# All six r scalings on VectorE, r's first scaling moved up in its slot, and the weight splits moved

## The reference, cut to what matters

```python
def _attn_ref(r, k, v, w, u):
    state = zeros(B, H, D, D)
    for t in range(S):
        cur = einsum('bhd,bhe->bhde', u * k[t], v[t])
        y[t] = einsum('bhd,bhde->bhe', r[t], state + cur)
        state = w[t][..., None] * state + einsum('bhd,bhe->bhde', k[t], v[t])

def _moe_ref(x, w_in, g_ln, w_sg, b_sg, w_out):
    h = gelu_tanh(x @ w_in)
    u, v = split(h)                      # halves of the columns
    v_n = layer_norm(v) * g_ln
    gated = u * (einsum('ts,bsd->btd', w_sg, v_n) + b_sg)
    return x + gated @ w_out

def _moe2_ref(x, mu_k, mu_r, w_k, w_v, w_r):
    xk, xr = mixes of x and x shifted by one step
    return sigmoid(xr @ w_r) * (relu(xk @ w_k) ** 2 @ w_v)
```

## Time and profile before

| | us |
|---|---|
| median of 3 runs (lowest, highest) | 423.65 (422.62, 425.02) |
| the profiled execution, its own time | 422.52 |
| its span | 420.8 |
| PE busy in the span | 368.8 (88%) |
| DVE busy | 260.1 (62%) |
| ACT busy | 182.2 (43%) |
| POOL busy | 125.0 (30%) |
| L565, r scalings on POOL, 24 instructions of 1762 ns | 42.2 |
| L870, r scalings on DVE, 16 of 1207 ns | 19.3 |
| L863, k scalings on DVE, 40 of 949 ns | 37.9 |
| L853, first_r on DVE, 16 of 569 ns | 9.1 |
| L1124, idle time of PE just before the w transposes | 22.6 |

### The profile page before, as it was taken

The page is one execution under the profiler, slowest core; times in us unless marked ns, Lnnn a source line. Parts: engine busy times, 40 slices in busy tenths (PEclk is TensorE's granted clock), DMA queues, the critical chain, the costliest instruction groups (busy, mean ns, idle before and its releaser), DMA issues.

```text
span 420.8 us, 9110 instructions
## 1 busy us (share of the span) xinstructions
PE 368.8 (88%) x3836; PEld 347.9 (83%) x3836; DVE 260.1 (62%) x380; ACT 182.2 (43%) x312; POOL 125.0 (30%) x141
## 2 busy tenths in 40 slices
PE   4656758879697899949999999999999999999997
PEld 3445647667596787849998999999999999999996
DVE  6467889797979983571645535998796311764011
ACT  3644627364554544543312406626783800565100
POOL 5936535271625732100000000520970000473000
PEclk9887869698888999959999999999999999999999
DMA  7997281716202101100100000305000011000011
GB/s 133 195 259 156 48 202 47 162 50 113 58 4 58 31 3 30 30 2 20 47 2 0 0 2 4 147 0 176 33 2 0 2 37 58 19 2 0 19 39 56
DMA packets 58840, 23.59 MB, mean 56 GB/s; under 512 B 52912, under 2 KB 56368, under 8 KB 58800
## 3 DMA queue, kind: packets, MB, share of 16 engines
q1 hardware_dynamic: 58800, 23.02, 22.1%
HBM read 18.29 MB, written 2.36 MB: 49 GB/s over the span
## 4 chain that ended last, share of the span: by engine, by line
PE 78%; issue 8%; ACT 6%; DVE 5%; SPq 1%; DMA 1%; POOL 0%; DVEq 0%; ACTq 0%; POOLq 0%
PE ps L1201 20%; PE ps L1202 19%; PE ps L1203 19%; PE ps L1192 4%; PE ps L1124 4%; PE ps L1188 3%; PE ps L1146 3%; PE ps L1134 2%; DVE kT L863 1%; PE ps L1157 1%; ACT ktok L651 1%; DVE sc L908 1%; PE ps L1129 1%; ACT rU L630 1%; ACT r L633 1%
## 5 line engine op out<-in xcount | busy, mean ns | idle before, releaser
L565 POOL TENSOR_TENSOR r<-r,wb 112x768 f32<-112x768 f32 x24 | 42.2, 1762 | 83.1 <-PE ps L1192 82.4
L613 POOL TENSOR_TENSOR sq_f<-sq_f 128x384 f32<-128x384 f32 x32 | 33.8, 1071 | 74.9 <-ACT sq_f L753 74.8
L863 DVE TENSOR_TENSOR kT<-kT,wb 112x384 f32<-112x384 f32 x40 | 37.9, 949 | 19.0 <-PE ps L1192 18.9
L1192 PE MATMUL ps<-r,kT 112*64 112x64 f32 x960 | 38.9, 238 | 7.1 <-DVE kT L863 4.3
L1192 PEld LDWEIGHTS ps<-r,kT 112*64 112x64 f32 x960 | 34.5, 150 | 12.7 <-issue 6.8
L1039 DVE TENSOR_TENSOR ot<-ps,ee 128x384 f32<-128x384 f32 x12 | 6.7, 558 | 54.6 <-PE ps L1203 54.6
L1024 DVE TENSOR_TENSOR sq_l<-sq_f,sq_h 128x384 fp32r<-128x384 f32 x32 | 27.7, 864 | 10.4 <-ACT sq_h L758 10.4
L1203 PE MATMUL ps<-xk_h,wk_l 128*128 128x384 f32 x96 | 32.2, 335 | 0.0
L1202 PE MATMUL ps<-xk_l,wk_h 128*128 128x384 f32 x96 | 32.2, 335 | 0.0
L1201 PE MATMUL ps<-xk_h,wk_h 128*128 128x384 f32 x96 | 32.2, 335 | 0.0
L1201 PE MATMUL ps<-wv_h,sq_h 128*128 128x384 f32 x96 | 32.1, 334 | 0.0
(11 more groups left out here) (146 smaller groups left out, 971.2 us busy)
## 6 DMA issues: line engine op xcount, KB each, us to landing
tok_w<-in_w_dram SPq DMA_DIRECT2D x16, 144.0 KB, 3.2
tok_k<-in_k_dram SPq DMA_DIRECT2D x16, 144.0 KB, 3.2
tok_r<-in_r_dram SPq DMA_DIRECT2D x16, 144.0 KB, 3.2
sgn<-in_moe_w_sg_dram SPq DMA_DIRECT2D x6, 384.0 KB, 3.9
vt<-in_v_dram SPq DMA_DIRECT2D x32, 72.0 KB, 2.6
out_dram<-ot SPq DMA_DIRECT2D x12, 192.0 KB, 1.9
xT<-yT SPq DMA_DIRECT2D x12, 144.0 KB, 2.6
win_raw<-in_moe_w_in_dram SPq DMA_DIRECT2D x1, 1536.0 KB, 7.5
```

Of the source, the lines that this page charges most:

```text
L565: nc.gpsimd.tensor_tensor(t, t, pair_of(h, 0, q).unsqueeze(1).unsqueeze(3).broadcast_to([ROWS, 2, S // (2 * h), h]), ALU.mult).then_inc(r_ ...
L613: nc.gpsimd.tensor_tensor(t, t, t, ALU.mult).then_inc(k_sq, 1)
L863: nc.vector.tensor_tensor(t, t, pair_of(h, 1, q).unsqueeze(2).broadcast_to([ROWS, S // (2 * h), h]), ALU.mult).then_inc(k_scaled, 1)
L1192: ins = nc.tensor.matmul(level_bank(l)[CHUNK[g], c * CH:(c + 1) * CH].rearrange("p (x t) -> p x t", x=2), kT[q % 4][0:ROWS, s], right2(r2[ ...
```

## The change

The level-3, level-4 and level-5 scalings of r leave GpSimd and stand in VectorE's list, each between scale_k and take_level of its level; GpSimd keeps the joins. Every wait on r_scaled_pool becomes one on r_scaled_dve. first_r and first_k are issued where their job stands in TensorE's order, so first_r comes after the old pair's level 5 and ahead of levels 3 and 1. low_sg and its semaphore go: ScalarE copies the sg transpose as plain fp32 to wsg_f (the same place as wsg_l), which alone frees the turn banks, and the six pieces of w_sg are split later from SBUF, cast by ScalarE in slots 15 to 18 and subtracted by VectorE in slots 16 to 19. The six w_in pieces move to slots 2 to 5 (cast) and 3 to 6 (low half), the three w_out pieces to slots 20 and 21. Up to slot 11 the low halves stand at the start of a slot, from slot 12 on after its levels and chain.

```diff
     for slot in range(SLOTS):
-        R_SCALES += [(q, l) for q, l in level_jobs(slot) if 0 < l < DVE_R]
         R_SCALES += [(q, 0) for kind, q, *_ in side_jobs(slot) if kind == "r"]
-    POOL_SCALES = [(q, l) for q, l in LEVEL_JOBS if l >= DVE_R]
+        R_SCALES += [(q, l) for q, l in level_jobs(slot) if l]
...
-    SPLITS = {2: ("in", 0), 3: ("in", 1), 4: ("in", 2), 5: ("in", 3), 6: ("in", 4), 7: ("in", 5),
-              15: ("out", 0), 16: ("out", 1), 17: ("out", 2)}
-    LOW_SLOTS = [3, 4, 5, 6, 7, 8, 20, 20, 21]
+    HIGH_SLOTS = {("in", 0): 2, ("in", 1): 2, ("in", 2): 3, ("in", 3): 4, ("in", 4): 4, ("in", 5): 5,
+                  ("sg", 0): 15, ("sg", 1): 16, ("sg", 2): 16, ("sg", 3): 17, ("sg", 4): 17, ("sg", 5): 18,
+                  ("out", 0): 20, ("out", 1): 20, ("out", 2): 21}
+    LOW_SLOTS = {("in", 0): 3, ("in", 1): 3, ("in", 2): 4, ("in", 3): 5, ("in", 4): 5, ("in", 5): 6,
+                 ("sg", 0): 16, ("sg", 1): 17, ("sg", 2): 17, ("sg", 3): 18, ("sg", 4): 18, ("sg", 5): 19,
+                 ("out", 0): 21, ("out", 1): 21, ("out", 2): 21}
...
@@ gpsimd @@
-            def scale_r(q, l):
-                h = 1 << l
-                pool.wait_ge(scores, level_at(q, l) + 1)
...
-                t = right2(r2[q % 5][0:ROWS, :, :], h)
-                nc.gpsimd.tensor_tensor(
-                    t, t, pair_of(h, 0, q).unsqueeze(1).unsqueeze(3).broadcast_to([ROWS, 2, S // (2 * h), h]),
-                    ALU.mult).then_inc(r_scaled_pool, 1)
...
             for slot in range(SLOTS):
-                for q, l in level_jobs(slot):
-                    if l >= DVE_R:
-                        scale_r(q, l)
                 for q, l in joins(slot):
                     join(q, l)
@@ scalar @@
-                    nc.scalar.copy(wsg_h[:, :, q * P:(q + 1) * P].rearrange("p (b j) t -> p b j t", b=2),
+                    nc.scalar.copy(wsg_f[:, :, q * P:(q + 1) * P].rearrange("p (b j) t -> p b j t", b=2),
...
+            def high_half(piece):
+                kind, n = piece
+                _, raw, hi = halves(piece)
+                if kind == "sg":
+                    act.wait_ge(copied, turn_at[("sg", C - 1)] + 1)
+                else:
+                    act.wait_ge(win_in if kind == "in" else wout_in, 16)
+                nc.scalar.copy(hi, raw).then_inc(w_high, 1)
...
+                for piece in PIECE_LIST:
+                    if HIGH_SLOTS[piece] == slot:
+                        high_half(piece)
@@ vector @@
-            def low_sg(n):
-
-                dve.wait_ge(copied, turn_at[("sg", n)] + 1)
...
             for slot in range(SLOTS):
+                for n, piece in enumerate(PIECE_LIST):
+                    if LOW_SLOTS[piece] == slot and slot < 2 * LEVELS:
+                        low_half(n)
                 for job in pe_jobs(slot):
                     if job[0] == "level":
                         q, l = job[1:]
                         if l:
                             scale_k(q, l)
-                        if 0 < l < DVE_R:
+                        if l:
                             scale_r(q, l)
                         take_level(q, l)
-                    elif job[0] == "sg":
-                        low_sg(job[1])
-                for job in side_jobs(slot):
-                    if job[0] == "k":
-                        first_k(job[1])
                     elif job[0] == "r":
                         first_r(job[1])
-                    elif job[0] == "u":
+                    elif job[0] == "k":
+                        first_k(job[1])
+                for job in side_jobs(slot):
+                    if job[0] == "u":
                         chain(job[1])
...
+                for n, piece in enumerate(PIECE_LIST):
+                    if LOW_SLOTS[piece] == slot and slot >= 2 * LEVELS:
                         low_half(n)
@@ tensor @@
-                elif last[0] == "sg":
-                    pe.wait_ge(sg_low, last[1] + 1)
...
-                    if l <= DVE_R:
-                        pe.wait_ge(r_scaled_dve, r_at(q, l - 1))
-                    else:
-                        pe.wait_ge(r_scaled_pool, pool_r_at(q, l - 1))
+                    pe.wait_ge(r_scaled_dve, r_at(q, l - 1))
...
-                        pe.wait_ge(sg_low, C)
+                        pe.wait_ge(w_low, split_at("sg"))
```

More of the change, by code:

```diff
@@ L115, in join_at @@
         return JOINS.index((q, l)) + 1
-    SPLITS = {2: ("in", 0), 3: ("in", 1), 4: ("in", 2), 5: ("in", 3), 6: ("in", 4), 7: ("in", 5),
-              15: ("out", 0), 16: ("out", 1), 17: ("out", 2)}
-    LOW_SLOTS = [3, 4, 5, 6, 7, 8, 20, 20, 21]
-    PIECES = len(SPLITS)
+    HIGH_SLOTS = {("in", 0): 2, ("in", 1): 2, ("in", 2): 3, ("in", 3): 4, ("in", 4): 4, ("in", 5): 5,
[4 more added lines that the diff above has]
+                 ("out", 0): 21, ("out", 1): 21, ("out", 2): 21}
+    PIECE_LIST = list(HIGH_SLOTS)
+    PIECES = len(PIECE_LIST)
     def split_at(kind):
-        return max(n + 1 for n, piece in enumerate(SPLITS.values()) if piece[0] == kind)
+        return max(n + 1 for n, piece in enumerate(PIECE_LIST) if piece[0] == kind)
     def segments(q):
@@ L171, in rwkv_gmlp_channel_mix_kernel @@
         wsg_l = at("wsg_l", [P, C, S], F32R, A_sg + SG)
+        wsg_f = at("wsg_f", [P, C, S], F32, A_sg + SG)
         A_out = A_sg + 2 * SG
@@ L403, in halves @@
                 return win_l[:, m, c], win_raw[:, m, c], win_h[:, m, c]
+            if kind == "sg":
+                return wsg_l[:, n, :], wsg_f[:, n, :], wsg_h[:, n, :]
             return [t.ap().rearrange("p f d -> p (f d)")[:, n * FH:(n + 1) * FH] for t in (wout_l, wout_raw, wout_h)]
@@ L542, in join @@
                         pool.wait_ge(k_scaled, k_at(q - 2, l + 1))
-                        if l + 1 < DVE_R:
-                            pool.wait_ge(r_scaled_dve, r_at(q - 2, l + 1))
-                        else:
-                            pool.wait_ge(r_scaled_pool, pool_r_at(q - 2, l + 1))
+                        pool.wait_ge(r_scaled_dve, r_at(q - 2, l + 1))
                     nc.gpsimd.tensor_tensor(blocks(q, 2 * h), pair_of(h, 0, q), pair_of(h, 1, q),
@@ L916, in low_half @@
             def low_half(n):
-                lo, raw, hi = halves(list(SPLITS.values())[n])
+                lo, raw, hi = halves(PIECE_LIST[n])
                 dve.wait_ge(w_high, n + 1)
                 nc.vector.tensor_tensor(lo, raw, hi.bitcast(F32), ALU.subtract).then_inc(w_low, 1)
-            def low_sg(n):
-                dve.wait_ge(copied, turn_at[("sg", n)] + 1)
-                c = slice(n * P, (n + 1) * P)
-                nc.vector.tensor_tensor(wsg_l[:, :, c].rearrange("p (b j) t -> p b j t", b=2),
-                                        turn[:, :, 0:HF].rearrange("p b (j t) -> p b j t", j=3),
-                                        wsg_h[:, :, c].bitcast(F32).rearrange("p (b j) t -> p b j t", b=2),
-                                        ALU.subtract).then_inc(sg_low, 1)
             def low_x(b, m):
@@ L1064, in _ @@
                         nc.vector.memset(aT[s][:, :, :, :], 0.0).then_inc(zeroed, 1)
-                for n in range(PIECES):
-                    if LOW_SLOTS[n] == slot:
+                for n, piece in enumerate(PIECE_LIST):
+                    if LOW_SLOTS[piece] == slot and slot >= 2 * LEVELS:
                         low_half(n)
@@ L1153, in y_job @@
                 pe.wait_ge(masked, level_at(q, LEVELS - 1) + 1)
-                pe.wait_ge(r_scaled_pool, pool_r_at(q, LEVELS - 1))
+                pe.wait_ge(r_scaled_dve, r_at(q, LEVELS - 1))
                 for n in range(1, NCH):
```

10 lines of the change are left out of this document (1 added, 9 removed).

## The result

| | before | changed |
|---|---|---|
| median, us (lowest to highest) | 424.33 (422.62 to 425.53) | 401.56 (400.33 to 402.79) |
| ratio, 95% interval | | 0.9466 (0.9417 to 0.9516) |
| profiled execution, its span | 420.8 | 398.7 |
| busy: PE, DVE, ACT, POOL | 368.8, 260.1, 182.2, 125.0 | 361.1, 259.8, 186.6, 87.2 |

The kernel is 22.8 us faster by the medians; 406.0 was forecast. VectorE is busy for as long as before, though it has taken over GpSimd's 24 multiplies.

The account below looks back on a forecast made before the run. VectorE and TensorE waiting for each other, through first_r's bank gate, were taken to bound the loop; 11.8 + 2.4 + 2.4 + 1.6 - 1.3 = 16.9 off 422.5 gives 405.6, median put at 406.0; range 401 to 417.

Parts of the forecast that it names:

- The bank gate and the low clock bound the kernel: Per period, TensorE's w transpose waits 2.08 us for first_r to free the turn banks, then runs slow at clock 0.85.
- the rival of the low clock: TensorE stays at slow prices and reaches the scan at 16.7 us, 1.7 above 15.0; time about 411.5, chance 0.20.
- VectorE's own work, 13.4 us a period: VectorE in one period: 12.3 us without GpSimd, less 1.5 for sg and w_in, plus 2.6 for three r scalings.
- Joins cost 1.2 and waits 0.35: Added to VectorE's 13.4 us for GpSimd's remaining joins and for waits, giving a period of 15.0 us.
- The rate of 0.42 us for each us of GpSimd: VectorE's stretch in the old period from 84.87: 3.4 us laid to GpSimd's 8.08 us busy.
- The rival of costly joins: GpSimd's joins cost VectorE their full length, up to 3.5 us, period 17.3; time about 414, chance 0.12.
- k waited for low_sg only another 0.5: On TensorE in the old period, k waited for low_sg until 101; freeing the sg transpose by ScalarE's copy saves 0.5 us.
- The stretch ahead of the first scan: 2.4 and 1.6: Gains of 2.4 us from 39.61 to 65.76 and 1.6 before 39.61, the latter bounded by 0 and 3.9.
- 1.3 us lost at the norm: Cost on the path of work not spread around the layer norm and of later ScalarE work; bounds 0 and 5.1.
- the cover: VectorE's 3.83 us wait for ScalarE at the norm's first low part, covering 3.5 us of work around the norm.
- VectorE slower through the contended price: Rival: moved scalings cost 2.27 us each whoever causes the long rows, period 20.2; time about 430, chance 0.08.
- The condition: The slower-VectorE rival decides from a period of 18.9 us on, that is from 5.5 us above 13.4.

Follow-up runs that it names:

- the fillers: Changed kernel with added GpSimd multiplies on a scratch tile in slots 7 to 14: 12 of 112x768 (long), 411.4 us, or 36 of 112x192 (short), 400.9 us.
- weights where they were: Changed kernel without its third part, w_sg split from PSUM in its own slot, w_in and w_out pieces where they were: 413 us by the ratio.
- after_again: The changed kernel itself, measured again beside the interleaved kernel: 402.2 us, ratio 0.9457.
- short fillers: Changed kernel with 36 added GpSimd multiplies of 112x192 on a scratch tile in slots 7 to 14: 400.9 us.
- ktok_first: Changed kernel with ScalarE's six casts of the normalised v behind the last pair's k transpose copy and wm copy: 399.8 us, ratio 0.9461.
- level 5 on GpSimd: Changed kernel with only level 5's scaling of r (8 of the 24) given back to GpSimd: 401.0 us, ratio 0.9467.
- the interleaved kernel: Changed kernel with last pair's k copy before the norm's casts, slot 20's gelus and state copy between them, last scan between norm steps: 392.5 us, ratio 0.9244.

## Why the prediction was right, and where it was not

The side was right and 401.56 lies near the low end of the range; the move was 22.8 us by the medians where 17.6 was forecast. The sum itself gave 405.6 for an execution like the profiled one and so 406.7 for the median; the 406.0 that was put down instead is not worked out. The low end of 401 stood on 13.9 us a period (measured 13.87) and no cost at the norm (measured 2.1). That the time comes within 0.6 of it all the same is in part luck: the early slots gave 1.8 more than their term and the stretch past the last u 0.6. By its steps:

- *The bank gate and the low clock bound the kernel.* The gate is shown: with first_r moved alone 14 us went and w follows kt at once. The clock over the three periods is 1.00 in that kernel and in the changed one, so the rival of the low clock does not hold. What the low clock cost by itself is not separated: with the scalings alone it rises to 0.97 and 12 us go though the gate stays. VectorE's stretched list was a limit beside the gate.
- *VectorE's own work, 13.4 us a period.* Right: 13.87 was measured, with VectorE full.
- *Joins cost 1.2 and waits 0.35.* This is the step that failed, by size: what is left beside 13.4 is 0.45, with no waits, and 0.33 of it is the one k multiply of 0.88. The rate of 0.42 us for each us of GpSimd came from long scalings, and the fillers show that short instructions do not cost it. Over the three periods it is the 3.4 us between 45.0 and 41.6. The rival of costly joins falls for the same reason.
- *k waited for low_sg only another 0.5.* The price fitted the old layout alone. In the new one the gate is 2.1 to 3.1 us a period, with the low clock behind it (weights where they were). The sum was not touched, since the change removes it; my picture of the third part as small was wrong.
- *The stretch ahead of the first scan: 2.4 and 1.6.* Measured 4.2 and 1.6, in one execution; the changed kernel reached the first scan 0.7 later in after_again. The early slots gain nearly a full period's gain in spite of the three low halves. That VectorE, at 21.40 of 21.97 busy, had no room left is shown; that the casts did not delay it is read from the trace, not tested.
- *1.3 us lost at the norm.* Measured 2.1, and for other reasons. The wait for ScalarE shrank from 3.83 to 1.17, so the cover held. What was lost is ahead of it: the u of slot 16 started 9.11 us behind the scan for 8.97 but ran at the low clock (2.47 for 1.48), and that of slot 18 waited 1.19 for its copy, behind two w_sg casts, for 0.81. With short fillers the first ran at 1.48 and the next u stood 25.6 us behind the scan, for 27.2 in the changed kernel and 25.3 before. Why the clock fell there stays open.
- *VectorE slower through the contended price.* The condition was never met: r multiplies average 974 ns.

What I had not seen at all is that the three parts are no sum. By the ratios, times 424 us, scalings alone give 11.6, first_r alone 13.2, the weights nothing; scalings with first_r 10.8, scalings with the weights 13.9, first_r with the weights 20.4; all three 22.6. Differences of 2 or 3 us between these are within the intervals, those of 6 and more are not. The parts take away three waits on one ring (the turn banks through first_r, the same banks through low_sg, VectorE's list), and the traces above show the next one in place when one is gone. Taken in the order first_r, weights, scalings, the third is worth 1 to 2 us, which the intervals do not tell from nothing; in the order scalings, first_r, weights, the weights are worth 12.

## What to carry to other kernels

Where several transposes share a PSUM bank, list every reader that frees it and where each stands in its engine's list; removing one gate is worth only the distance to the next, so price the parts together and in every order. A stretched VectorE multiply cost nearly nothing where its engine had slack (402.5 for 401.6), and 12 us where it had none (scalings alone). Look also at the list of an engine that is not busy: moving one copy ahead of six casts, and setting what waits behind it between them, was worth 9.7 us more by the medians.

## What the runs showed that was not expected

The cost of GpSimd beside VectorE went by the length of its instructions: VectorE was busy 1.7, 1.8 and 2.1 us longer a period than in the changed kernel (13.76) with 4.4 to 4.9 us more of GpSimd in pieces of 1.5 us or longer, and 0.8 to 1.0 longer with 5.9 us more in pieces of 0.5.

Early code that is the same, or nearly so, ran at different granted clocks in the first 30 us and reached the first scan at different times. The clock was 0.77 in both profiled executions of the changed kernel (first scan at 59.99 and 60.72) and with both fillers (61.47 long, 58.59 short, none of which stands ahead of that scan), 0.94 in ktok_first and in level 5 on GpSimd (57.49 and 57.71), and 0.89 in the interleaved kernel (59.08). The two fastest had the highest clock, but the clock alone does not settle it, for at 0.77 the scan came anywhere from 58.59 to 61.47. Those are up to 4.0 us whose cause stays open, so single executions of this kernel are not to be compared closer than that.
